# Payload rows of 64 products instead of 32 weights and two gates, in a fused softmax-mixture and top-2 expert kernel

## The reference

```python
    c = logits - logits.max(1, keepdims=True)
    c = np.exp(c)
    c /= c.sum(1, keepdims=True) + 1e-09
    return (c @ slot_out).astype(np.float32)
```

```python
    top2_w = np.exp(top2_l)
    top2_w /= top2_w.sum(-1, keepdims=True) + 1e-09
    for e in range(E):
        for k in range(2):
            mask = top2[:, k] == e
            h = np.maximum(x[mask] @ w1[e], 0.0)
            out[mask] += top2_w[mask, k, None] * (h @ w2[e])
```

## Time and profile before

| | us |
|---|---|
| median of 3 runs | 973.6 |
| lowest and highest run | 973.33, 973.91 |
| the profiled execution | 979.98 |
| its span, first to last instruction | 978.1 |
| TensorE busy in it | 905.8 (93%) |
| VectorE busy | 625.6 (64%) |
| ScalarE busy | 452.3 (46%) |
| GpSimd busy | 341.7 (35%) |

### The profile page before, as it was taken

The page is one execution under the profiler, slowest core; times in us unless marked ns, Lnnn a source line. Parts: engine busy times, 40 slices in busy tenths (PEclk is TensorE's granted clock), DMA queues, the critical chain, the costliest instruction groups (busy, mean ns, idle before and its releaser), DMA issues.

```text
span 978.1 us, 26085 instructions
## 1 busy us (share of the span) xinstructions
PE 905.8 (93%) x7930; PEld 726.2 (74%) x7931; DVE 625.6 (64%) x1398; ACT 452.3 (46%) x971; POOL 341.7 (35%) x362
## 2 busy tenths in 40 slices
PE   5999989996787679999999999999999999999995
PEld 5999979993463337878777777777777777777774
DVE  5132343346478968888776777677767777777773
ACT  2222221231041445555565666566656655665563
POOL 5000000001001022433455555555555656565652
PEclk9999989998656689999999999999999999999998
DMA  7447777887645212333333333333334444444441
GB/s 238 130 130 219 205 247 199 258 282 203 192 112 135 97 44 81 95 94 98 107 109 111 108 111 106 111 109 110 107 109 109 115 106 110 104 111 113 109 116 30
DMA packets 76908, 129.07 MB, mean 132 GB/s; under 512 B 10764, under 2 KB 45532, under 8 KB 74936
## 3 DMA queue, kind: packets, MB, share of 16 engines
q1 hardware_dynamic: 60696, 110.35, 38.3%
q0 software_dynamic: 15248, 17.49, 8.8%
q10 hardware_dynamic: 912, 0.52, 0.2%
HBM read 63.49 MB, written 16.86 MB: 82 GB/s over the span
## 4 chain that ended last, share of the span: by engine, by line
PE 87%; DVE 4%; DMA 4%; issue 2%; ACT 1%; POOL 0%; another core or an unknown queue 0%; ACTq 0%; SPq 0%; PEldq 0%; DVEq 0%
PE ps L1494 31%; PE ps L1498 15%; PE ps L1473 11%; PE ps L1229 10%; PE ps L1278 4%; PE ps L1280 4%; PE ps L1448 3%; PE ps L1222 3%; PE ps L1463 2%; DMA a_room<-in_moe_w 1%; PE ps L1375 1%; DMA lg<-in_moe_w 1%; PE ps L1394 1%; PE ps L1322 1%; DMA gate_room<-in_moe_w 1%
## 5 line engine op out<-in xcount | busy, mean ns | idle before, releaser
L681 ACT ACTIVATE x_ring<-ps 128x512 f16<-128x512 f32 x472 | 256.3, 598 | 215.3 <-PE ps L1473 188.2
L1494 PE MATMUL ps<-w2hl,x_ring 128*128 x1888 | 347.3, 327 | 1.1 <-DVE x_ring L1172 0.8
L1162 DVE SCALAR_TENSOR_TENSOR x_ring<-ps,x_ring 128x512 f16<-128x512 f32 x472 | 303.1, 684 | 11.5 <-ACT x_ring L681 5.1
L1494 PEld LDWEIGHTS ps<-w2hl,x_ring 128*128 128x128 f16 x1888 | 176.4, 97 | 97.8 <-issue 7.4
L553 POOL DMA_INDIRECT stage<-pay_rows,row_id x151 | 150.3, 995 | 275.9 <-PE ps L1473 159.2
L1498 PE MATMUL ps<-w2hl,x_ring 128*128 x1888 | 194.6, 246 | 1.1 <-DVE x_ring L1162 1.1
L563 POOL DMA_INDIRECT out_rows<-x_ring,row_id x151 | 169.8, 1125 | 58.4 <-issue 43.9
L1498 PEld LDWEIGHTS ps<-w2hl,x_ring 128*128 128x128 f16 x1888 | 163.1, 98 | 31.9 <-DVE x_ring L1162 1.9
L1473 PE MATMUL ps<-c,x_ring 96*128 96x128 f16 x1888 | 145.6, 220 | 0.5 <-DVE c L1155 0.5
L1155 DVE COPY c<-ps 96x256 f16<-96x256 f16 (+1 forms) x151 | 39.0, 258 | 143.7 <-PE ps L1463 124.8
L1473 PEld LDWEIGHTS ps<-c,x_ring 96*128 96x128 f16 x1888 | 122.6, 98 | 0.9 <-issue 0.9
(11 more groups left out here) (310 smaller groups left out, 658.6 us busy)
## 6 DMA issues: line engine op xcount, KB each, us to landing
x_ring<-a_room SPq DMA_DIRECT2D x236, 192.0 KB
x_ring<-in_x SPq DMA_DIRECT2D x14, 1536.0 KB, 6.9
stage<-in_moe_w SPq DMA_DIRECT2D x24, 768.0 KB, 9.6
a_room<-in_moe_w SPq DMA_DIRECT2D x12, 768.0 KB, 11.5
gate_room<-in_moe_w SPq DMA_DIRECT2D x8, 768.0 KB, 10.1
stage<-pay_rows,row_id POOLq DMA_INDIRECT x151
out_rows<-x_ring,row_id POOLq DMA_INDIRECT x151
pay_rows<-x_ring SPq DMA_DIRECT2D x1, 1904.0 KB, 6.0
```

What stands on the lines that cost most here:

```text
L681: a.activation(hh[:, m % 2, 4 * half:4 * half + 4, :].rearrange("p j q -> p (j q)"), ps[:, 2 + 2 * (m % 2) + half, :], ACT.Relu).then_inc( ...
L1162: last = v.scalar_tensor_tensor(hl[:, m % 2, 4 * half:4 * half + 4, :].rearrange("p j q -> p (j q)"), ps[:, 2 + 2 * (m % 2) + half, :], 0. ...
L1494: t_.matmul(ps[:, 6 + b % 2, 0:2 * D], hh[:, m % 2, j, :], w, start=k == 0 and j == 0, stop=False)
```

## The change

The payload row of a token now holds 64 numbers (256 bytes): the 32 combine weights times the first gate, and the same 32 times the second. GpSimd makes them with two multiplications over all rows, `c_gated[0]` in the x ring and `c_gated[1]` in place in `lg`. ScalarE's copy to `cg` and its semaphore are gone. SyncE writes the two halves of the payload rows as each is ready, so in DRAM each of the two transfers has 14336 pieces of 128 bytes. Since `lg` stays in use, the w1 loads that went there go to the room of `a3`, and the first of them waits for the slot experts' last product (`so_ps`) in place of `cg_ready`. In the block stage the split has no multiplication left: ScalarE rounds both passes' weights in one instruction, and VectorE subtracts in one.

```diff
-    KP = NS + 2
+    KP = 2 * NS
...
-        zero16 = sb("zero16", [P, 2 * NB], F16)
+        zero16 = sb("zero16", [P, 2 * 4 * KP], F16)
...
-        cg = ring[:, 0:T * KP].rearrange("p (t k) -> p t k", k=KP)
+        c_all_rows = lg[:, PAD:PAD + T, :]
+        c_gated = [ring[:, 0:T * NS].rearrange("p (t s) -> p t s", s=NS), c_all_rows]
...
-                    stage2[:, 0:2 * F], lg[:, :, :].rearrange("p t s -> p (t s)")[:, 0:2 * F]]
+                    stage2[:, 0:2 * F], a3_room[:, :].bitcast(F32)[:, 0:2 * F]]
...
+        def gated_rows(b):
+
+            at = slice(0, KP) if is_pair(b) else slice((1 - list_no(b)) * NS, (2 - list_no(b)) * NS)
+            return crow[:, b % CR, at].rearrange("p (k s) -> p k s", s=NS)
...
-                elif n == 2 * E + 2:
+                elif n in (2 * E + 2, 2 * E + 3):
                     sp.wait_ge(so_ps, E)
-                elif n == 2 * E + 3:
-                    sp.wait_ge(cg_ready, 1)
...
-            sp.wait_ge(cg_ready, 1)
-            sp.wait_ge(gates_ready, 2)
-            sp.dma_start(pay[0:N, :].rearrange("(p t) k -> p t k", t=T), cg[:, :, :]).then_inc(pay_out, 16)
+            for k in range(2):
+                sp.wait_ge(gates_ready, k + 1)
+                sp.dma_start(pay[0:N, k * NS:(k + 1) * NS].rearrange("(p t) s -> p t s", t=T), c_gated[k]
+                             ).then_inc(pay_out, 16)
...
             pool.wait_ge(sot_ps, 1)
+            pool.wait_ge(c_ready, 1)
...
-                g.tensor_tensor(cg[:, :, NS + k], pr[:, 3, :], pr[:, 4, :], ALU.add).then_inc(gates_ready, 1)
+                step(g.tensor_tensor(gm[:, 4 + k, :], pr[:, 3, :], pr[:, 4, :], ALU.add))
+                g.tensor_tensor(c_gated[k], c_all_rows, gm[:, 4 + k, :].unsqueeze(2).to_broadcast([P, T, NS]), ALU.mult
+                                ).then_inc(gates_ready, 1)
                 pool.wait_ge(gates_ready, k + 1)
...
-            act.wait_ge(sot_ps, 1)
-            a.activation(cg[:, :, 0:NS], lg[:, PAD:PAD + T, :], ACT.Copy).then_inc(cg_ready, 1)
...
-                for k in (range(2) if is_pair(b) else range(1)):
-                    gate = NS + (k if is_pair(b) else 1 - list_no(b))
-                    last = a.activation(csp[:, b % 4, k, 0:2, :],
-                                        crow[:, b % CR, 0:NS].unsqueeze(1).to_broadcast([P, 2, NS]), ACT.Copy,
-                                        scale=crow[:, b % CR, gate:gate + 1])
-                last.then_inc(cs_hi, 1)
+                n = 2 if is_pair(b) else 1
+                a.activation(csp[:, b % 4, 0:n, 0:2, :], gated_rows(b).unsqueeze(2).to_broadcast([P, n, 2, NS]), ACT.Copy
+                             ).then_inc(cs_hi, 1)
...
-                for k in (range(2) if is_pair(b) else range(1)):
-                    gate = NS + (k if is_pair(b) else 1 - list_no(b))
-                    last = v.scalar_tensor_tensor(csp[:, b % 4, k, 2, :], crow[:, b % CR, 0:NS],
-                                                  crow[:, b % CR, gate:gate + 1], csp[:, b % 4, k, 0, :],
-                                                  ALU.mult, ALU.subtract)
-                last.then_inc(cs_lo, 1)
+                n = 2 if is_pair(b) else 1
+                v.tensor_tensor(csp[:, b % 4, 0:n, 2, :], gated_rows(b), csp[:, b % 4, 0:n, 0, :], ALU.subtract
+                                ).then_inc(cs_lo, 1)
...
-    pay = nc.dram_tensor("pay_rows", (n + 512, 34), _mybir.dt.float32, kind="Internal").ap()
+    pay = nc.dram_tensor("pay_rows", (n + 512, 64), _mybir.dt.float32, kind="Internal").ap()
```

More of the change, by code:

```diff
@@ L287, in soft_then_top2_moe @@
         gate_inv, gates_ready = sem("gate_inv"), sem("gates_ready")
-        cg_ready, pay_out = sem("cg_ready"), sem("pay_out")
+        pay_out = sem("pay_out")
         cs_hi, cs_lo = sem("cs_hi"), sem("cs_lo")
@@ L437, in _ @@
                          zero16[:, 0:2 * 4 * KP].bitcast(F32)).then_inc(zero_rows, 16)
-            sp.wait_ge(cg_ready, 1)
-            sp.wait_ge(gates_ready, 2)
-            sp.dma_start(pay[0:N, :].rearrange("(p t) k -> p t k", t=T), cg[:, :, :]).then_inc(pay_out, 16)
+            for k in range(2):
+                sp.wait_ge(gates_ready, k + 1)
+                sp.dma_start(pay[0:N, k * NS:(k + 1) * NS].rearrange("(p t) s -> p t s", t=T), c_gated[k]
+                             ).then_inc(pay_out, 16)
             sp.wait_ge(eid_ready, 4)
             sp.wait_ge(a3_in, 16 * 12)
-            sp.wait_ge(pay_out, 16)
+            sp.wait_ge(pay_out, 32)
             def copy_a(i, m):
@@ L566, in _ @@
             pool.wait_ge(zero_rows, 16)
-            pool.wait_ge(pay_out, 16)
+            pool.wait_ge(pay_out, 32)
             pool.wait_ge(tab_ready, 2)
```

## The result

| | before | changed |
|---|---|---|
| median of 7 runs, us | 973.6 | 981.77 |
| lowest and highest run | 973.33, 976.03 | 978.71, 986.73 |
| the profiled execution | 979.98 | 983.24 |
| its span | 978.1 | 981.4 |

The changed kernel takes 1.0082 times as long, with a 95% interval of 1.0057 to 1.0107. That is 8.2 us more; the forecast was 10.9 more, 984.5 us. Three later comparisons put the changed kernel, rebuilt without an edit or with edits that turned out to do nothing, at 1.0063 to 1.0077. So the loss is 6 to 8 us. In the list of experiments each kernel has a label, e1 to e15.

A forecast was written before the change was run, and what follows sets the result against it. TensorE bounds the block stage, and the chain ahead of it runs on VectorE, which GpSimd's products hold. 979.98 + 11.4 - 0.5 = 990.9 us profiled; the same 10.9 us on 973.6 give 984.5 us, range 979 to 1000.

The forecast's parts named there:

- The sign and the place: Slower, chance 0.86: GpSimd's products hold VectorE on the chain ahead of the lookups, shifting the block stage 11.4 us.
- The price of a product: GpSimd's multiplication over 3584 elements per partition: 8.0 us each, lower end 3.3, upper end 13.4.
- The prediction's own timetable: First product 313.97 to 321.97 us, second 323.5 to 331.5; L1014 moves from 320.49 to 331.85, a shift of 11.4 us.
- other gains of 0.5 us: Shorter splits, visible at the block stage's entry (about 0.2 us) and two chain places (0.15 each): together -0.5 us.
- Which instruction is caught: First product holds VectorE's cast L996 (or L998), some 8 us; L1006 passes beside the second, L1014 waits some 3 us.
- ScalarE's copy: Copy of the weights, 3.21 us at 269.56, goes; ScalarE idles afterwards until 278.5, so worth nothing.
- the moved w1 load: Fourth late load of the gate experts' w1 issues at about 268.5 us instead of 272.80; worth nothing.
- the gathers of 256 bytes: Block-stage gathers fetch 256 bytes a row instead of 136; ScalarE waited for gathers only three times, so nothing.
- The payload: Two writes of 14336 pieces each, 11 to 20 ns a piece, down by 360 us before the 370.2 us gather; cost nothing.
- The first, that VectorE loses almost nothing: Rival at the products: long GpSimd instructions let VectorE in between, costing 0.25 us; total 973.3 us; chance 0.14.
- The second, that L1006 is held: Rival: the seven multiplications from PSUM wait for the second product too; shift 15.8, total 988.9 us; chance 0.10.
- The third, the late payload: Rival at the payload writes: 34 ns a piece, landing at 385 us, 15 us more, total 999.4 us; chance 0.18.

The follow-up runs named there:

- e1: Changed kernel once more, unedited: 980.75 us, 1.0065 of the kernel before.
- e15: The kernel before, unedited, on the third comparison's chip: 977.1 us, 0.9997 of before.
- e2: Changed kernel without GpSimd's two products, both payload halves written from the bare weights: 974.68 us, 1.0002 of the kernel before.
- e6: Changed kernel with both products over only the first 56 of 112 tokens of each partition: 977.45 us, 1.0028 of the kernel before.
- e12: Changed kernel with VectorE waiting for the second gate, then a small copy ahead of its last count instruction, so the second product starts first: 990.17 us, 1.0132 of before.
- e8: Changed kernel with each pair's split again two instructions on ScalarE and two on VectorE, each with a multiplication by one: 984.32 us, 1.0075 of before.
- e9: Changed kernel with the second product released by a VectorE signal ahead of its last but one count instruction; nothing was caught: 984.6 us, 1.0077 of before.
- e13: Changed kernel, unedited, on the third comparison's chip: 984.2 us, 1.0063 of the kernel before.
- e5: Changed kernel with GpSimd's second product also waiting until VectorE's counts are done: 981.49 us, 1.0067 of the kernel before.
- the first comparison: Changed kernel again, without products, with the second product later, and with half products, beside the kernel before at 974.3 us.
- the second's: Second comparison: kernel before again, and changed kernel with two-instruction splits, catch by signal, or earlier gates, beside the kernel before at 977.07 us.
- the third's: Third comparison: changed kernel with catch by order, unedited, or with products shared, and the kernel before again, beside the kernel before at 978.12 us.
- e14: Changed kernel with early exponential; VectorE computes the first gate and product, GpSimd only the second product, behind VectorE's counts: 980.81 us, 1.0031 of before.

## Why the prediction came out as it did

**The sign and the place were right.** The chain runs over VectorE between 310 and 330 us, and GpSimd's long instructions stop VectorE there. e2 takes the products out and the loss is gone. e6 halves them and the held cast halves to the same hundredth. e12 moves one instruction into a product's shadow and pays 6 us.

**The price of a product was mis-sized.** The forecast took 8.0 us from the slope of 112-element multiplications (2.18 ns an element); measured are 6.23 us for 3584 and 3.21 for 1792, 1.69 ns an element and 0.19 us besides. That line gives 0.38 us for 112 elements, where the rows have 0.42: the 0.04 us between them, divided by 112 and taken times 3584, is most of the error. A small rest in one short row became a large one at 32 times the size. The prediction's own timetable says shift = two products less 4.64 us. With 6.23 that is 7.8 us. In the narrower stretch e1, e8, e9 and e13, in that order of events, show 7.7 against the profile that the timetable was built on, and 6.9 against the other two of the kernel before. With the other gains of 0.5 us the sum would have said 7.3 us more; these runs and e5 took 6.1 to 7.5 more. Two products too dear by 1.77 us each make 3.5 us, which covers the gap to the 8.2 measured and more. The estimate of 7.9 us scaled from the Trainium skill (GPSIMD Engine Reference, Elementwise — side-by-side cycle accounting) does not agree with the trace either. Its figure is for an addition; here it is a multiplication with one operand repeated 32 times, and no run shows what makes the difference.

**Which instruction is caught was taken as fixed.** The prediction named L996 or L998 as the first victim and let the second product meet the PSUM multiplications. In the first profiled execution it met L1004 (the kernel before's L1001) instead, and the local delay was 11.5 us in place of 8: near the forecast's 11.4, but by another way. That agreement of numbers is chance. How often each order comes in the changed kernel is not settled: one of the five profiled executions of it without an effective edit (first, e1, e8, e9, e13) had the catch. The first seven runs lie 8.0 us apart (978.71 to 986.73), those of e1, e8, e9 and e13 1.4 to 3.3 us. Both orders among the seven would look like that, but only one of them has a profile.

**Other gains of 0.5 us**: the size can't be told from nothing (e2: 0.4 us the other way, within 1.1). ScalarE's copy, the moved w1 load and the gathers of 256 bytes were put at nothing, and e2, which has them all, agrees. ScalarE's split took 0.31 us instead of the 0.40 forecast, VectorE's 0.23 with 0.25 forecast, both without effect: e8.

**The payload was priced right.** 11 to 20 ns a piece were forecast. From 322 to 332 us 13594 pieces passed in 10 us, by 16 engines 11.8 ns each; a single one took 19.4 ns, with more than one in progress per engine (164.6% of 160 us). The writes were down at 339 us; the forecast had them down by 360 and needed them by 370. e2, which writes the same pieces, costs nothing.

**The rivals.** The first, that VectorE loses almost nothing, fell by the 6.23 us rows. The second, that L1006 is held, fell by e1. The third, the late payload, fell by the 28 us to spare.

**A step that misled after the result.** The two first profiles differed by 4.9 us behind the first gather and by 3.6 us ahead of `slot_out` (269.56 against 266.01), and I first read a gain into that. The kernel before's profiled execution was 6.4 us above its median. Over all profiled executions the last stretch took 614.4 to 619.9 us, with no tie to the splits: 616.3 with the short ones in e2, 617.9 and 618.6 in e13 and e9, 618.6 with the long ones in e8. Part of it goes with the chip: 614.8 to 616.3 us on that of the first comparison, 618.0 to 618.6 on the second's, 617.9 to 619.9 on the third's. Why stays open, and so does the difference between the two first profiles.

## What to carry to other kernels

Work moved to an idle GpSimd is not free where VectorE is on the critical path: in these executions a VectorE instruction on SBUF alone that came due during a product on GpSimd (a copy, a cast, a `tensor_scalar`, one with two inputs) stood until the product's end, and those with an operand in PSUM passed, so long instructions belong beside VectorE's reads of PSUM, its waits, or after its chain. Work taken off engines that follow a busy TensorE (here 29 us of ScalarE) bought nothing to pay with. Where two engines' instructions start within some hundredths of a microsecond of each other, look at several executions before explaining a total.

## What was unexpected of the hardware

- A start order of 0.03 or 0.04 us between the two engines moves the chain by 4.6 us (16.94 to 21.54 in the narrower stretch): L1004 started 0.03 us behind a product and was held 6.24 us; in e1 it ended 0.04 us ahead of one and took 0.43.
- A held instruction can be tiny. The cast that waited 6.23 us wrote 28 numbers of one partition, and L1014 (28 partitions, 85 numbers) waited 1.89 us.
- VectorE is held by GpSimd's short steps too, and so falls into step with it: small count instructions that take 0.17 to 0.22 us in e14, where GpSimd is idle beside them, show 0.38 to 0.47 elsewhere and end within 0.08 us of GpSimd's. In the first profile L551 had started 0.01 us ahead of the two scans (308.82 and 308.83). With the scans at 0.98 us instead of 0.54, VectorE was one instruction behind when the first product began, and that decided which one was caught.
- A product of 3584 numbers per partition takes 4.08 us on VectorE and 6.23 us on GpSimd. Where GpSimd's holds VectorE for its whole length, moving the product to GpSimd costs VectorE 2 us instead of saving 4.
